# Routing tables and the running count of a fused attention and mixture kernel, and the form of its last output tile

## The reference, cut to what matters

```python
x = attention(q, k, v)       # 8 heads, local and dilated windows
x = mixture_1(x)             # 4 attention experts, the best 2 of each token, causal
# mixture_2: 8 feed-forward experts, one for each token
logits = x @ w_gate                        # (B, S, 8)
local_gate = sigmoid(x @ w_local)          # (B, S)
for b in range(B):
    prev_e = -1
    for s in range(S):
        fresh_e = argmax(logits[b, s])
        e = fresh_e if s == 0 or local_gate[b, s] < 0.5 else prev_e
        prev_e = e
        p = softmax(logits[b, s])
        h = maximum(x[b, s] @ w1[e], 0)
        out[b, s] = p[e] * (h @ w2[e])
```

## Time and profile before

| | us |
|---|---|
| median of 3 runs | 748.64 |
| lowest and highest | 747.83 and 752.16 |
| profiled execution, its own time | 744.36 |
| its span in the profile, first to last instruction | 742.6 |
| mean granted TensorE clock of the span | 0.987 |

### The profile page before, as it was taken

How to read it: one execution, slowest core, us unless ns; L and a number is a source line. 1 busy time by engine, 2 the same in 40 slices (tenths; PEclk the granted TensorE clock), 3 DMA queues, 4 the chain that set the end, 5 groups by cost and what they waited for, 6 DMA issues and landing times.

```text
span 742.6 us, 15648 instructions
## 1 busy us (share of the span) xinstructions
PE 720.8 (97%) x5297; PEld 532.6 (72%) x5298; DVE 309.3 (42%) x935; ACT 287.3 (39%) x848; POOL 100.7 (14%) x149
## 2 busy tenths in 40 slices
PE   8999999999999989997999899999999999999997
PEld 8987766786677866774674667777776777777674
DVE  3762788258861788414537511121121112112111
ACT  3661678336862578412340032123213212321320
POOL 4300001000000001000002311121121112112213
PEclk9999999999999999997899999999999999999999
DMA  7486128212451214100006215271061571100101
GB/s 170 100 198 146 37 58 218 71 42 50 115 155 49 64 26 142 58 8 0 15 30 248 71 30 191 82 262 41 28 241 56 194 291 54 42 28 28 50 28 37
DMA packets 86517, 69.72 MB, mean 94 GB/s; under 512 B 69118, under 2 KB 69150, under 8 KB 86464
## 3 DMA queue, kind: packets, MB, share of 16 engines
q1 hardware_dynamic: 78816, 44.73, 21.4%
q0 software_dynamic: 7648, 24.29, 9.8%
HBM read 118.12 MB, written 11.27 MB: 174 GB/s over the span
## 4 chain that ended last, share of the span: by engine, by line
PE 92%; DVE 4%; ACT 2%; issue 1%; another core or an unknown queue 1%; POOL 0%; DVEq 0%; ACTq 0%; POOLq 0%
PE bank L1105 21%; PE bank L1116 20%; PE bank L766 9%; PE bank L762 5%; PE bank L840 5%; PE bank L691 4%; PE bank L806 4%; PE bank L674 4%; PE bank L828 4%; PE bank L731 3%; PE bank L783 3%; PE bank L704 2%; PE bank L667 2%; PE bank L663 1%; PE bank L1088 1%
## 5 line engine op out<-in xcount | busy, mean ns | idle before, releaser
L1105 PEld LDWEIGHTS bank<-pt,stage_b 128*128 128x128 f32 x1344 | 155.0, 192 | 10.0 <-issue 10.0
L1116 PE MATMUL bank<-w_all,raw_all 128*128 x352 | 158.2, 592 | 0.0
L1105 PE MATMUL bank<-pt,stage_b 128*128 128x128 f32 x1344 | 156.9, 275 | 0.0
L1468 ACT ACTIVATE raw_all<-bank 128x512 f32<-128x512 f32 x44 | 26.3, 597 | 216.4 <-PE bank L1105 216.4
L1116 PEld LDWEIGHTS bank<-w_all,raw_all 128*128 128x128 f32 x352 | 63.6, 190 | 63.6 <-issue 63.6
L1939 DVE TENSOR_SCALAR raw_all<-bank,p_slot 128x512 f32 x21 | 15.8, 751 | 209.2 <-PE bank L1116 209.2
L617 POOL DMA_INDIRECT out_dram<-raw_all,idx_out x25 | 37.6, 1506 | 250.4 <-DVE raw_all L1939 233.5
L766 PE MATMUL bank<-stage_b,w_all 128*128 128x288 f32 x256 | 67.6, 411 | 0.1
L1294 ACT ACTIVATE pr<-sm,negmax_a 96x80 f32<-96x80 f32 (+1 forms) x168 | 59.7, 359 | 2.2 <-DVE negmax_a L1516 2.0
L766 PEld LDWEIGHTS bank<-stage_b,w_all 128*128 128x128 f32 x256 | 46.7, 190 | 13.7 <-issue 2.7
L1283 ACT COPY w_sb<-bank 128x256 f32<-128x256 f32 (+5 forms) x93 | 38.7, 420 | 42.6 <-PE bank L806 41.1
(11 more groups left out here) (223 smaller groups left out, 911.6 us busy)
## 6 DMA issues: line engine op xcount, KB each, us to landing
w_sb<-in_moe_w_dram SPq DMA_DIRECT2D x19, 2048.0 KB
w_all<-in_moe_w_dram SPq DMA_DIRECT2D x19, 2048.0 KB
w_sb<-in_moe_w_dram POOLq DMA_DIRECT2D x12, 512.0 KB, 4.8
w_all<-in_moe_w_dram POOLq DMA_DIRECT2D x12, 512.0 KB, 5.1
raw_all<-in_q_dram SPq DMA_DIRECT2D x32, 144.0 KB
raw_all<-in_k_dram SPq DMA_DIRECT2D x32, 144.0 KB
mixture_rows<-y_sb SPq DMA_DIRECT2D x16, 256.0 KB, 2.7
v_dil<-in_v_dram SPq DMA_DIRECT2D x42, 80.0 KB, 2.9
```

What stands on the lines that cost most here:

```text
L1105: last = pe.matmul(ps[half][:, f * P:(f + 1) * P], w1_sb[:, 0, c * F + at:c * F + at + P] if buf is None else w1_fix[:, c, at:at + P], xT[ ...
L1116: last = pe.matmul(ps[5], hidT[:, half * HALF + n * P:half * HALF + (n + 1) * P], w2_sb[:, bass.ds(buf, 1), half, n * D:(n + 1) * D].rearr ...
```

## The change: what it does, and the diff

1. The output projection of the 64-token tile is computed as two column tiles: rows 0 to 63 of the bank take the first 256 output columns, rows 64 to 127 the other 256, each with a matmul for each pair of experts. The copy is then 128x256, and the store is two DMAs of 64 rows by 256 columns.
2. In routing the padding of the sequence is -1 instead of 0, so that no expert matches there; the multiplication with c_valid and the constant go. The one-hot table lies expert by expert (chosen), with a zero column ahead and one behind for each expert.
3. The running count over the tiles (upto) is a scan on VectorE over the one-hot table itself, ahead of the product with ones, which is now added in PSUM to the product with the triangle. Its last column is each expert's total.
4. The token's number goes onto the one-hot rows (low_token, is_equal and mult in one instruction for each of the 20 tiles) instead of onto reach; token_hot goes.
5. The probability table: VectorE makes the difference of reach and, in the same 20-instruction form, low_prob, which takes the place of low_token. GpSimd's two instructions go.
6. Fillers on TensorE: 5 wide ones instead of 8 behind the counting products, three of 128 columns ahead of each second and third chunk, 3 wide ones instead of 2 ahead of the second set of products, and 1 instead of 2 behind it.
7. Two waits on the slots' tables are split: buffers_ready after the table of buffers, table_ready at the end. Seven table operations move into dve_route_late. TensorE waits for buffers_ready only ahead of its first output product, behind both halves of the first hidden layer.

```diff
@@ store_y
             n = TILE[t]
+            w = D * n // P
             sp.wait_ge(y_moved[t % 2], b * CNT2[t % 2] + t // 2 + 1)
-            sp.dma_start(xs[bass.ds(b * S + T0[t], n), :], y_sb[t % 2][0:n, :]).then_inc(y_stored[t % 2], 16)
+            for r in range(0, P, n):
+                c0 = r // n * w
+                sp.dma_start(xs[bass.ds(b * S + T0[t], n), c0:c0 + w], y_sb[t % 2][r:r + n, 0:w]
+                             ).then_inc(y_stored[t % 2], 16)
@@ gpsimd
-            pool.wait_ge(route_ready, 5)
-            pool.wait_ge(low_hot_ready, (LT + HOT - 1) // HOT)
-            pool.tensor_tensor(prob_hot, reach[:, :, 0:SLOTS], reach[:, :, 1:SLOTS + 1], ALU.subtract).then_inc(hot_step, 1)
-            pool.wait_ge(hot_step, 1)
-            pool.wait_ge(prob_ready, 1)
-            pool.tensor_tensor(prob_hot, prob_hot, r1[4][:, :].unsqueeze(2).broadcast_to([P, LT, SLOTS]),
-                               ALU.mult).then_inc(prob_hot_ready, 1)
...
@@ pe_out
+            n = D * nq // P
             for p in range(PAIR_E):
-                last = pe.matmul(X[0:nq, :], OT[:, p, T0[t]:T0[t] + nq], wo_sb[:, p, :],
-                                 start=(p == 0), stop=(p == PAIR_E - 1))
+                for r in range(0, P, nq):
+                    c0 = r // nq * n
+                    last = pe.matmul(X[r:r + nq, 0:n], OT[:, p, T0[t]:T0[t] + nq], wo_sb[:, p, c0:c0 + n],
+                                     start=(p == 0), stop=(p == PAIR_E - 1))
@@ tensor, routing
-            oh = heads_out[:, 0:LT * EF]
-            pe.wait_ge(pt2_moved, B * 2 * UNITS)
-            pe.matmul(ps[5][:, 0:LT * EF], ones[:, :], oh, start=True, stop=True)
-            pe.matmul(ps[3][:, 0:LT * EF], lower[:, :], oh, start=True, stop=True).then_inc(route_product, 1)
-            turn_wide(8)
-
-            pe.wait_ge(token_hot_ready, 1)
+            count = ps[3][:, 0:EF * (LT + 1)].rearrange("x (e t) -> x e t", e=EF)
+            pe.matmul(count, lower[:, :], chosen[:, :, 1:LT + 2], start=True, stop=False)
+            product(5)
+            pe.matmul(count, ones[:, :], upto[:, :, 0:LT + 1], start=False, stop=True).then_inc(route_product, 1)
+            turn_wide(5)
+
+            pe.wait_ge(reach_ready, 1)
             for t in range(LT):
                 r, g = divmod(t, FOLD)
                 if t % HOT == 0:
-                    pe.wait_ge(low_hot_ready, t // HOT + 1)
-                last = pe.matmul(ps[7][g * FW:g * FW + SLOTS + 1, 0:P], token_hot[:, t, :], low_hot[:, t, :],
+                    turn_over(pe, ps[0], 3 if t > 0 else 0)
+                    pe.wait_ge(low_token_ready, t // HOT + 1)
+                last = pe.matmul(ps[7][g * FW:g * FW + SLOTS + 1, 0:P], reach[:, t, :], low_token[:, t, :],
                                  start=(r == 0), stop=(t + FOLD >= LT))
...
-            turn_wide(2, 0)
-            pe.wait_ge(prob_hot_ready, 1)
+            turn_wide(3, 0)
             for t in range(LT):
                 r, g = divmod(t, FOLD)
-                last = pe.matmul(ps[6][g * FW:g * FW + SLOTS, 0:P], prob_hot[:, t, :], low_hot[:, t, :],
+                if t % HOT == 0:
+                    turn_over(pe, ps[0], 3 if t > 0 else 0)
+                    pe.wait_ge(low_prob_ready, t // HOT + 1)
+                last = pe.matmul(ps[6][g * FW:g * FW + SLOTS, 0:P], prob_hot[:, t, :], low_prob[:, t, :],
                                  start=(r == 0), stop=(t + FOLD >= LT))
...
-            turn_wide(2, 0)
+            turn_wide(1, 0)
             turn_x(0, True)
             turn_wide(1, 1)
             hidden(0, 0, None)
-            pe.wait_ge(table_ready, 1)
-            b0 = weights_of(0)
             turn_x(1)
             hidden(0, 1, None)
+            pe.wait_ge(buffers_ready, 1)
+            b0 = weights_of(0)
             output(0, 0, b0, True)
@@ dve_route
-            step(v_.memset(seq[:, S:NT * P], 0.0))
-            step(v_.memset(by_e[:, :, 0:1], 0.0))
+            step(v_.memset(seq[:, S:NT * P], -1.0))
+            step(v_.memset(chosen[:, :, :], 0.0))
...
+            tell(v_.tensor_tensor(rows_of.rearrange("x e (b t) -> x e b t", t=NT), took,
+                                  c_expert[:, :].unsqueeze(2).unsqueeze(2).broadcast_to([P, EF, B, NT]), ALU.is_equal))
+            tell(v_.tensor_tensor_scan(upto.rearrange("x e t -> x (e t)"), c_restart[:, :, :].rearrange("x a b -> x (a b)"),
+                                       chosen.rearrange("x e t -> x (e t)"), 0.0, ALU.mult, ALU.add))
             dve.wait_ge(route_product, 4)
...
+            tt(fillc[:, :, :], count[:, :, LT:LT + 1].broadcast_to([P, EF, TPW]), over(c_fill[:, :], EF), ALU.is_gt)
+            red(e8[0][:, :], fillc[:, :, :], ALU.add)
+            step(v_.tensor_tensor_scan(e8[1][:, :], ones[:, 0:EF], e8[0][:, :], 0.0, ALU.mult, ALU.add))
+            tt(e8[2][:, :], e8[1][:, :], e8[0][:, :], ALU.subtract)
+
+            stt(in_expert, along(e8[2][:, :], LT), float(P), count[:, :, 0:LT], ALU.mult, ALU.add)
+            tt(in_expert, in_expert, rows_of, ALU.mult)
+            red(r1[0][:, :], in_expert.rearrange("x e t -> x t e"), ALU.add)
+            v_.tensor_tensor(reach, along(r1[0][:, :], SLOTS + 1), over(c_slot[:, :], LT), ALU.is_ge).then_inc(reach_ready, 1)
...
+            for t in range(LT):
+                ins = v_.tensor_scalar(low_token[:, t, :], c_row[:, :], r1[1][:, t:t + 1], c_token[:, t:t + 1],
+                                       ALU.is_equal, ALU.mult)
+                if t % HOT == HOT - 1 or t == LT - 1:
+                    ins.then_inc(low_token_ready, 1)
...
             v_.tensor_copy(idx[:, 0, :], idx_f[:, 0, :]).then_inc(row_ready, 1)
 
+            dve.wait_ge(reach_ready, 1)
+            v_.tensor_tensor(prob_hot, reach[:, :, 0:SLOTS], reach[:, :, 1:SLOTS + 1], ALU.subtract).then_inc(prob_step, 1)
+            dve.wait_ge(prob_step, 1)
+            for t in range(LT):
+                ins = v_.tensor_scalar(low_prob[:, t, :], c_row[:, :], r1[1][:, t:t + 1], r1[4][:, t:t + 1],
+                                       ALU.is_equal, ALU.mult)
+                if t % HOT == HOT - 1 or t == LT - 1:
+                    ins.then_inc(low_prob_ready, 1)
...
-            step(v_.tensor_copy(tab_i[0:1, 0, :], tab[0:1, 1, :]))
+            v_.tensor_copy(tab_i[0:1, 0, :], tab[0:1, 1, :]).then_inc(buffers_ready, 1)
+            dve.wait_ge(buffers_ready, 1)
```

More of the change, by code:

```diff
@@ L172, in build @@
         r8 = [carve(heads_out, i * LT * EF, LT, EF) for i in range(12)]
+        chosen, upto = (carve(heads_out, (5 + 2 * i) * LT * EF, EF, LT + 2) for i in range(2))
         Vf = V[:, :, :].rearrange("x a b -> x (a b)")
@@ L183, in build @@
         c_later = sb("c_later", [P, LT])
-        c_valid = sb("c_valid", [P, LT])
-        c_restart = sb("c_restart", [P, EF, LT + 1])
+        c_restart = sb("c_restart", [P, EF, LT + 2])
         r1 = [sb(f"r1_{i}", [P, LT]) for i in range(6)]
@@ L535, in _ @@
             select(later_v[:, :, 0], [[0, B]], 0, 1, ALU.not_equal, 0.0)
-            fill(c_valid[:, :], 1.0)
-            valid_v = c_valid[:, :].rearrange("x (b t) -> x b t", t=NT)
             for t in range(NT):
@@ L1273, in move_y @@
                 return
-            nq = TILE[t]
+            n = D * TILE[t] // P
             eng.wait_ge(y_done, m * NT + t + 1)
-            n = m * CNT2[t % 2] + t // 2
-            if n > 0:
-                eng.wait_ge(y_stored[t % 2], 16 * n)
-            copy(y_sb[t % 2][0:nq, :], X[0:nq, :]).then_inc(y_moved[t % 2], 1)
+            stored = m * STORES[t % 2] + t // 2
+            if stored > 0:
+                eng.wait_ge(y_stored[t % 2], 16 * stored)
+            copy(y_sb[t % 2][:, 0:n], X[:, 0:n]).then_inc(y_moved[t % 2], 1)
         def act_copy(o, i):
@@ L1477, in _ @@
             first_slots(1)
+            act.wait_ge(table_ready, 1)
+            used = slots_used(act)
             end = last_slot(act)
@@ L1756, in over @@
                 return a.unsqueeze(1).broadcast_to([a.shape[0], m, a.shape[1]])
-            one_hot, ex, dd, t3, t4 = r8[0], r8[1], r8[2], r8[3], r8[4]
-            by_e, upto = (carve(heads_out, (5 + 2 * i) * LT * EF, EF, LT + 1) for i in range(2))
+            ex, dd, t3, t4 = r8[1], r8[2], r8[3], r8[4]
+            in_expert = carve(heads_out, 0, EF, LT)
+            rows_of = chosen[:, :, 1:LT + 1]
             logits = LG[:, :, 0:EF]
@@ L1793, in dve_route @@
[L1793 to L1799 removed]
+            took = ps[4][:, 0:LT].rearrange("x (t b) -> x b t", b=B).unsqueeze(1).broadcast_to([P, EF, B, NT])
@@ L1868, in over @@
                 return a.unsqueeze(1).broadcast_to([a.shape[0], m, a.shape[1]])
+            ts(tab[0:1, 2, :], tab[0:1, 0, :], float(NBUF), ALU.add, float(EF - 1), ALU.min)
+            step(v_.tensor_copy(tab_i[0:1, 1, :], tab[0:1, 2, :]))
+            ts(tab[0:1, 2, :], tab[0:1, 0, :], float(EF - NBUF) - 0.5, ALU.is_lt)
+            step(v_.memset(tab[0:1, 3, :], 0.0))
```

(3 more changed lines are left out.)

62 lines of the change are left out of this document (17 added, 45 removed).

## The result

The change makes the kernel slower: 755.73 us, median of 20 executions (748.68 to 766.32), against 747.62 for the kernel before beside it (20 executions, 740.37 to 754.71). The ratio after to before is 1.0105, 95% interval 1.0071 to 1.0138.

The account below looks back on a forecast made before the run. TensorE, busy 97% of the span, was taken as the bound. Tiles 2.7 plus routing 0.2 gave 2.9 us off 744.36, so 741.5; plus 4.3 to the runs' median, 745.7 us, with an 8-in-10 range of 742.0 to 749.8.

Parts of the forecast that it names:

- the sum's last: Whole kernel: profiled execution forecast at 741.5 us; the runs' median kept 4.3 above it, giving 745.7 us.
- Rival 1: Routing: TensorE's waits for tables drop the clock to 1.2 GHz early; +3.4 us, 749.1 us, chance 0.16.
- The output tile: Attention's last output tile: halves run side by side, 0.96 instead of 1.86 us; three tiles count, 2.7 us saved.
- Rival 4: Last output tile: the two array halves don't overlap, only 0.2 us is won; 748.4 us, chance 0.08.
- VectorE starts again behind the counting products: Routing: VectorE resumes at 398.7 as before; change 0, between -0.3 and +0.3 us.
- Each series of 20: Routing's tables on VectorE: 20 operations of 128x128 at 0.256 us each, 5.1 us; bounds 3.0 and 6.9.
- rival 3: Routing's tables: each VectorE operation takes half of 0.256 us, hidden layer 3.4 us earlier; 742.3 us, chance 0.10.
- The third chunk of products: Routing on TensorE: the last chunk of token table products starts at 407.9 us, against 407.81 before.
- The gather: Routing: starts at 410.8 us, takes 0.6 longer beside VectorE's table operations, which nobody waits for.
- rival 2: Routing: GpSimd starves, the gather gets through only when VectorE's series ends; +1.4 us, 747.1 us, chance 0.08.
- The probability tables: Routing on VectorE: ready at 415.9 us, where before they were ready at 410.2.
- "no change" in routing: Routing as a whole: first hidden layer at 419.6 us against 419.78 before, counted as 0.2 us gained.

Follow-up runs that it names:

- the first fillers: Filler matmuls in TensorE's idle places in attention, except ahead of position 8's scores: added to the kernel before, 744.87 us; with the new output tile alone, 742.13 us.
- with all: Filler matmuls also ahead of position 8's scores: added to the kernel before, 744.45 us; to the kernel before with the new output tile alone, 739.54 us.
- all three filled kernels: Kernel after, kernel before, and kernel before with the new output tile alone, each with filler matmuls except ahead of position 8's scores: 745.50, 744.87, 742.13 us.

## Why the prediction was wrong

**The step that failed** is the sum's last: "The median of the runs shown, 748.64, lies 4.3 above it; I keep that difference". That difference is not a constant beside the work but the granted clock's, and the change moved it. The profiled execution of before took 744.36, below all three of the runs then known (747.83 to 752.16), and had no fall in its three attention periods: it was a lucky one. In the batch of 35, five executions of before took 744.3 or less, at a clock of 0.987 or more, and those at 0.981 took about 749. I priced work against the lucky one and never asked what the other executions lose, nor what a different output tile does to it. Measured, the lost time went from 16.8 (15.4 in another batch) to 26.4 us, about +10 and rough, since the batches differ. The work went down by 3.4 (1.9 against the other batch), and the median moved by +8.1.

A second, smaller part may lie in the base. The 20 executions of before beside the result have a median of 747.62, like the batch whose times are those without the stall and not like the two at 750.8. If they had no stall, routing was longer by some 3.5 us there. Their clocks are not on record, so this stays open.

**Rival 1 had the right mechanism in the wrong place.** It let the clock fall early in routing, by routing's gaps. In the profile after, the clock stays up through its waits of 1.61 and 0.46 us and falls only at 434, and the whole of routing at that clock is 1.5 us longer than at full clock. The falls that decided begin at 100, 192 and 284, in the attention periods, behind gaps of 0.20 to 0.47 that the prediction does not list. I also held "each gap is under 1.9" against the rival; size of the single gap was no argument. The Trainium skill has a case of this kind in "TensorE: Matmul & The Clock Gate", section "A second HAM failure mode: psum-queue depth-cycling": a bf16 kernel in which TensorE pauses only briefly between groups of matmuls, and its clock goes down and up again all the same. These traces agree (idle 0.20 to 0.47 us, then 0.50), and add that the same pauses do it in one execution and not in another.

**The output tile: right.** Forecast 2.7 us for three tiles, at 0.96 each; in the chain they take 1.01, which saves 0.85 each. Between kernels that differ in it alone, at a clock of 0.999 or more: 737.13 - 734.40 = 2.7 with the first fillers, 739.02 - 736.63 = 2.4 with all. Both pairs are of one batch. Rival 4 (halves don't overlap) is out.

**Routing, term by term, from the last copy of the logits (390.72 before, 410.24 after).** VectorE starts again behind the counting products at +7.92, forecast +8.0. Each series of 20 takes 5.21 us, forecast 5.1; rival 3, and with it the estimate of 0.13 us per operation from "VectorE: DVE Perf Modes" of the Trainium skill, is out at a measured 0.26. The third chunk of products starts at +17.1, forecast +17.2. The subtraction without GpSimd beside it takes 0.19, forecast 0.2. The gather takes 1.23 beside VectorE's series where I allowed 1.07 + 0.6; rival 2 is out. The probability tables end at +25.1, forecast +25.2. The hidden layer starts at 29.0 at full clock, forecast 28.9. The chain has VectorE's second series and no unknown source, as written.

**But "no change" in routing rested on a stall, as the prediction said of itself.** "5 us of new VectorE work cost nothing only because a 2.2 us stall, a low clock and some fillers go". The 29.06 us of the old routing held both the stall and the low clock behind it. At full clock the old routing takes 27.4 us with the stall and 25.5 without, and the new one 28.99: it is 1.6 or 3.5 us slower, where the sum has it 0.2 faster. Of the parts tried, the fastest executions are those of the new tile with the old routing and the fillers (734.40 and 736.63, against 737.84 and 737.96 with the new routing).

## What to carry to other kernels

A profile is one execution: before working out microseconds, compare its time and its mean clock with the other executions, and look at what separates them; here that was 10 us against 3 of work. In a kernel that TensorE bounds, a change that takes work off a period can cost more clock than it saves. The test is cheap: put matmuls on the identity into the small idle places of the period and look at the slowest executions, not only the fastest. When an edit is free only because a stall of unknown origin goes, price it against the kernel without that stall too. And before a stall is put down to a program, compare an unchanged kernel across the batches at the same clock.

## What the runs showed of the hardware

- Idle times of 0.2 to 0.5 us in an engine busy 97% of the time were followed by 1.2 GHz for 16 to 18 us in some executions and not in others, at a cost of about 7 us each. With an idle 0.38 ahead of the scores of position 8 left open, all three filled kernels had a fall right behind it in their profile; with it filled, none of four had one in these periods.
- The same program spread over 17.6 us (748.68 to 766.32), in steps, with its granted clock; with fillers over 5.6 us (737.96 to 743.55).
- Issuing a product twice moved the median by -6.5 us against the kernel after, and issuing it three times by +5.4 (different batches). Why was not settled: the falls recur, are spared and recur, and no run here set the length of the period without adding work.
- The copy behind the second fold product waits 2.2 us longer than its product in five profiles of the old routing and not in two. By the times of the unchanged kernel this seems to go with the batch and not with the program; 24 more instructions on ScalarE left it where it was.
